# Softmax weights times v in three fp32r passes, divisors inverted in transposed 32x32 blocks, and a new order of the engines in attention

## The reference

```python
q_bits = (q @ proj > 0); k_bits = (k @ proj > 0)        # 6 bits per token
mask   = q_bucket[:, :, :, None] == k_bucket[:, :, None, :]
scores = where(mask, q @ k.T / 8, -1e9);  scores -= scores.max(-1)
attn   = exp(scores);  attn = attn / (attn.sum(-1) + 1e-9)
x = (attn @ v) as [1536, 512]
h = maximum(x @ w_in, 0);  x = h * h @ w_out            # 512 -> 2048 -> 512
# routing: tokens to 8 experts, 192 each, by descending logits of x @ w_gate
out[chosen by e] = maximum(x @ w1[e], 0) @ w2[e]        # 512 -> 1024 -> 512
```

## Time and profile before

| | us |
|---|---|
| median of 3 executions | 868.71 (867.45 to 880.04) |
| the profiled execution | 874.02 |
| its span, first to last instruction | 872.3 |
| attention in it, about | 24 to 309 |
| first layer | 309 to 590 |
| routing and experts | 590 to 872 |

### The profile page before, as it was taken

How to read it: one execution, slowest core, us unless ns; L and a number is a source line. 1 busy time by engine, 2 the same in 40 slices (tenths; PEclk the granted TensorE clock), 3 DMA queues, 4 the chain that set the end, 5 groups by cost and what they waited for, 6 DMA issues and landing times. The chain is left out here.

```text
span 872.3 us, 13757 instructions
## 1 busy us (share of the span) xinstructions
PE 816.2 (94%) x4688; PEld 703.0 (81%) x4688; DVE 416.4 (48%) x885; ACT 321.6 (37%) x575; POOL 283.4 (32%) x284
## 2 busy tenths in 40 slices
PE   5999999999999999999999999995399899999996
PEld 3776777767776778899989989994299899999996
DVE  7566666666666565242232224223644354455410
ACT  1344434444344555454554554440012122122221
POOL 3122312223122367655665566651100201110101
PEclk8899999999999999999999999996589999999999
DMA  7355546667545200010000001000344443635451
GB/s 170 73 116 117 126 91 131 139 144 173 136 96 138 88 1 0 0 37 1 0 36 0 0 0 37 0 1 36 115 150 159 166 178 129 217 134 208 136 208 36
DMA packets 65763, 81.28 MB, mean 93 GB/s; under 512 B 41304, under 2 KB 41304, under 8 KB 65216
## 3 DMA queue, kind: packets, MB, share of 16 engines
q1 hardware_dynamic: 63680, 74.54, 31.2%
q0 software_dynamic: 2048, 6.29, 2.2%
HBM read 54.55 MB, written 6.29 MB: 70 GB/s over the span
## 5 line engine op out<-in xcount | busy, mean ns | idle before, releaser
L586 PE MATMUL banks<-pt,v_raw 128*128 128x384 f32 x384 | 150.6, 489 | 0.0
L324 ACT ACTIVATE pt<-banks 128x768 f32<-128x768 f32 x96 | 77.9, 812 | 139.7 <-PE banks L536 138.5
L887 DVE TENSOR_TENSOR h<-relu 128x384 f32<-128x384 f32 x64 | 42.9, 670 | 174.0 <-ACT relu L842 174.0
L728 POOL TENSOR_TENSOR wi_lo<-w_in_sb,wi_hi 128x512 fp32r<-128x512 f32 x64 | 83.9, 1312 | 102.7 <-ACT wi_hi L721 101.6
L408 DVE TENSOR_REDUCE mx<-banks 128x1 f32<-128x768 f32 x96 | 91.7, 957 | 26.2 <-PE banks L563 23.3
L1406 PE MATMUL banks<-x_cols,w_in_sb 128*128 128x192 f32 x512 | 97.3, 343 | 1.3 <-ACT x_cols L1186 1.1
L1420 PE MATMUL banks<-expert_hidden,w_out_sb 128*128 128x192 f32 x512 | 94.6, 335 | 0.0
L732 POOL TENSOR_TENSOR wo_lo<-w_out_sb,wo_hi 128x512 fp32r<-128x512 f32 x64 | 84.7, 1323 | 15.1 <-ACT wo_hi L724 15.1
L1406 PEld LDWEIGHTS banks<-x_cols,w_in_sb 128*128 128x128 f32 x512 | 85.9, 198 | 3.8 <-issue 2.1
L962 PE MATMUL banks<-xt_hi,wi_hi 128*128 128x384 f32 (+1 forms) x256 | 86.4, 337 | 0.0
L962 PE MATMUL banks<-xt_lo,wi_hi 128*128 128x384 f32 (+1 forms) x256 | 86.0, 336 | 0.0
(11 more groups left out here) (181 smaller groups left out, 1288.7 us busy)
## 6 DMA issues: line engine op xcount, KB each, us to landing
w_in_sb<-in_moe_w SPq DMA_DIRECT2D x8, 2048.0 KB, 9.7
w_out_sb<-in_moe_w SPq DMA_DIRECT2D x8, 2048.0 KB, 8.1
w_in_sb<-in_moe_w_in SPq DMA_DIRECT2D x8, 512.0 KB, 6.1
w_out_sb<-in_moe_w_out SPq DMA_DIRECT2D x8, 512.0 KB, 5.1
w_out_sb<-in_k SPq DMA_DIRECT2D x16, 192.0 KB, 3.8
w_out_sb<-in_q SPq DMA_DIRECT2D x16, 192.0 KB, 3.9
v_raw<-in_v SPq DMA_DIRECT2D x16, 192.0 KB, 3.7
kb<-k_hi SPq DMA_DIRECT2D x16, 192.0 KB
```

The lines of the kernel that those rows point to most:

```text
L324: act.activation(halves(pt[j % 2]), both(ST), ACT.Exp, scale=SCALE).then_inc(ex, 1)
L586: last = pe.matmul(O[:, h, 0:HALF], v_raw[i][:, j, :], pt[j % 2][:, h * HALF:(h + 1) * HALF], start=False, stop=j == 5)
L728: pool.tensor_tensor(wil[i][:], in_view(f), wih[i][:].bitcast(fp32), ALU.subtract).then_inc(wils, 1)
```

## The change

- `weighted` goes. ScalarE makes pt_hi (fp32r) from pt in SBUF (`expo_high`), VectorE or GpSimd make pt_lo = pt - pt_hi (`low_part`: tiles 0 to 3 of the even head and 0, 1, 3 of the odd one on GpSimd, the other five on VectorE). v is split the same way (`v_high` on ScalarE, `v_low_part` on GpSimd). TensorE does v_hi x pt_hi, v_lo x pt_hi (`weigh_high`) and v_hi x pt_lo (`weigh_low`), each in fp32r for both halves.
- VectorE takes O out of PSUM whole (`take`, two halves), turns the divisor rows to the other partitions with a transpose in 32x32 blocks (`turn`), inverts one column per block (128x24) and spreads it by a second transpose (`invert`). GpSimd's `divide` is two operations of 64x768.
- The orders of all five engines are new; expo(j) waits for the low part that was read from its buffer, not for a matmul. v is loaded without padding and later; the weight loads of two heads stand together; GpSimd's first three weight splits stand behind the last divide.
- k_hi and the like share their memory with the weight splits of the first layer. The four reciprocals in the first chunk of that layer go.

```diff
-        v_raw = [sb(f"v_raw{i}", [P, TT, P]) for i in range(2)]
+        v_raw = [sb(f"v_raw{i}", [P, TT, D]) for i in range(2)]
+        def low_part(eng, i, p, j):
+            n = 2 * p + i
+            eng.wait_ge(his, 6 * n + j + 1)
+            if past(6 * n + j, 2):
+                eng.wait_ge(pvl, 6 * n + j - 1)
+            eng.tensor_tensor(pt_lo[j % 2][:], pt[j % 2][:], pt_hi[j % 2][:].bitcast(fp32), ALU.subtract).then_inc(los[i][j], 1)
...
SyncE, per pair:
+                asm_kb(2 * p + 1, 1)
+                part_ka(1)
+                asm_qb(2 * p + 1, 1)
+                part_qa(1)
+                more_q(p + 2)
+                if p + 1 < PAIRS:
+                    load_v(2 * p + 2, 0)
+                if p:
+                    load_v(2 * p + 1, 1)
+                weights(2 * p)
+                weights(2 * p + 1)
+                if p + 1 < PAIRS:
+                    asm_kb(2 * p + 2, 0)
+                    asm_qb(2 * p + 2, 0)
+                more_k(p + 2)
+                if p + 1 < PAIRS:
+                    part_ka(0)
+                    part_qa(0)
...
GpSimd:
             def divide(g):
                 pool.drain()
-                pool.wait_ge(num_, 2 * g + 1)
+                pool.wait_ge(evac, 4 * g + 2)
+                pool.wait_ge(rec, g + 1)
+                for i in range(2):
+                    pool.drain()
+                    pool.tensor_tensor(rden[VSL[i], :], nd[i][VSL[i], :], rden[VSL[i], :], ALU.mult).then_inc(nrm, 1)
...
+            for p in range(PAIRS):
+                if p:
+                    free_row(2 * p - 1, 1)
+                low_part(pool, 0, p, 0)
+                low_part(pool, 0, p, 1)
+                low_part(pool, 0, p, 2)
+                sum_v(2 * p + 1, 1)
+                low_part(pool, 0, p, 3)
+                if p:
+                    low(p - 1)
+                if p + 1 < PAIRS:
+                    free_row(2 * p, 0)
+                    sum_v(2 * p + 2, 0)
+                v_low_part(2 * p + 1, 1)
+                low_part(pool, 1, p, 0)
+                low_part(pool, 1, p, 1)
+                low_part(pool, 1, p, 3)
+                divide(p)
+                if p + 1 < PAIRS:
+                    v_low_part(2 * p + 2, 0)
+            split["in_low"](pool, 0, 0, 0)
+            split["in_low"](pool, 1, 1, 1)
+            split["out_low"](pool, 0, 0, 0)
             low(PAIRS - 1)
...
ScalarE:
             def expo(n, j):
                 act.wait_ge(st, 6 * n + j + 1)
+                if j > 1:
+                    act.wait_ge(los[n % 2][j - 2], n // 2 + 1)
+                elif n:
+                    act.wait_ge(los[(n - 1) % 2][j + 4], (n - 1) // 2 + 1)
+            def expo_high(n, j):
+                act.wait_ge(ex, 6 * n + j + 1)
                 if 6 * n + j > 1:
+                    act.wait_ge(pvh, 6 * n + j - 1)
+                act.activation(pt_hi[j % 2][:], pt[j % 2][:], ACT.Copy).then_inc(his, 1)
...
VectorE:
+            def take(n, i, h, divided):
+                dve.wait_ge(pvh, 6 * n + 6)
+                dve.wait_ge(pvl, 6 * n + 6)
                 if past(divided, 1):
                     dve.wait_ge(nrm, 2 * divided)
+                dve.tensor_copy(nd[i][:, h * HALF:(h + 1) * HALF], O[:, h, 0:HALF]).then_inc(evac, 1)
+            def turn(n, i):
+                dve.wait_ge(evac, 2 * n + 2)
+                dve.transpose(turned[VSL[i], :], nd[i][VSL[1 - i], :])
+            def invert(rows, free, done):
+                dve.drain()
+                dve.tensor_scalar(divisor[rows, :], turned[rows, :].rearrange("p (b c) -> p b c", c=SQ)[:, :, 0], GUARD, None, ALU.add)
+                dve.drain()
+                dve.reciprocal(divisor[rows, :], divisor[rows, :])
+                dve.drain()
+                dve.transpose(rden[rows, :].rearrange("p (b c) -> p b c", c=SQ),
+                              divisor[rows, :].unsqueeze(2).broadcast_to([rows.stop - rows.start, S // SQ, SQ])).then_inc(done, 1)
+            def pair(p, first, last):
+                if not first:
+                    low_part(dve, 1, p - 1, 5)
+                    take(2 * p - 1, 1, 0, p)
+                    take(2 * p - 1, 1, 1, p)
...
+                max_done(2 * p + 1)
+                low_part(dve, 0, p, 4)
+                if not first:
+                    turn(2 * p - 1, 1)
+                low_part(dve, 0, p, 5)
+                v_low(2 * p + 1, 1)
+                take(2 * p, 0, 0, p)
+                take(2 * p, 0, 1, p)
+                    row_max(2 * p + 2, 0)
+                turn(2 * p, 0)
+                    row_max(2 * p + 2, 1)
+                    row_max(2 * p + 2, 2)
+                    row_max(2 * p + 2, 3)
+                low_part(dve, 1, p, 2)
+                    row_max(2 * p + 2, 4)
+                    row_max(2 * p + 2, 5)
+                    max_done(2 * p + 2)
+                invert(EVERY, p, rec)
+                low_part(dve, 1, p, 4)
+                    v_low(2 * p + 2, 0)
...
TensorE (the new order of one pair, shortened; s_t = scores_t, s = scores of the next head):
+            def weigh_high(i, p, j):
+                if j == 0:
+                    pe.wait_ge(vls, n + 1)
+                pe.wait_ge(his, 6 * n + j + 1)
+                for v_ in (v_hi[i], v_lo[i]):
+                    for h in range(2):
+                        last = pe.matmul(O[:, h, 0:HALF], v_[:, j, :], pt_hi[j % 2][:, h * HALF:(h + 1) * HALF], start=False, stop=False)
+                last.then_inc(pvh, 1)
+            def weigh_low(i, p, j):
+                pe.wait_ge(los[i][j], p + 1)
...
```

501 lines of the change are left out of this document (253 added, 248 removed).

## The result

The changed kernel takes 885.26 us (median of 4 executions, 883.35 to 886.46) against 868.82 (4 executions) before: a ratio of 1.0155, 95% interval 1.0082 to 1.0228. I had predicted 858 with a range of 840 to 882; it is slower, by 0.8 to 2.3 per cent, and outside the range. The two profiled executions have spans of 881.6 and 872.3 us, 9.3 us apart. The medians are 16.4 us apart. The traces can explain the 9.3. The mean granted clock goes with this spread: of 82 executions of the kernel before on the four chips of the experiments, those under 870 us have clocks of 0.964 to 0.971 and those over 874.5 us 0.958 to 0.962; the profiled one has 0.961. So before's trace is that of an execution with a low clock.

The account below looks back on a forecast made before the run. TensorE was taken to bound the eight attention pairs. Seven pairs -11.5, last pair -1.5, hand-over +2, copies +1 and start +0.3 gave about -10 us, so 858 from the median of 868.7, range 840 to 882.

Parts of the forecast that it names:

- Pairs 2 to 7: Steady attention pairs: 34.6 us each instead of 36.25, predicted as -9.9 us for these six.
- the start: Start of the kernel, ahead of the first pair: four memsets for two, +0.3 us.
- The saving of the three passes: TensorE, per pair: 72 fp32r matmuls replace 24 fp32 ones, 2.9 us less, stream from 33.7 to 30.8 us.
- the first rival: Only TensorE and q count; GpSimd's divide and lows slip into idle time: pair 33.3 us, whole 849; chance 0.33.
- The chain ahead of scores_t(even, 3): First half of a pair: 12.4 us of GpSimd-led work beside 9.0 of TensorE; stall 2.9 us after overlap.
- The second half of the pair: Waits of 0.4 us at the next head's scores and 0.6 at weigh_low(even, 5): 1.0 us.
- The port rival: VectorE's low_parts each wait for a whole GpSimd operation: pair 40.1 us, whole 897; chance 0.14.
- The last pair: Last attention pair, without preparation: chain near 2 us per tile, gives back 1.5 of 30.0 us.
- The hand-over: Attention to first layer: in_low stands behind the last divide, about 2.5 us late, costing 2 us.
- The copies: kb and qb copies by SyncE: hidden but tight, 0 to 3 us in the whole, taken as +1.
- The clock: TensorE's lower busy share lowers its clock; a tenth of the stream at 1.2 GHz adds 25 us: 883; chance 0.05.
- ScalarE, VectorE and GpSimd: Work per pair: from 15.7, 24.4 and 9.1 us to 25, 27.9 and 26.

Follow-up runs that it names:

- without contention and divide: Changed kernel, divide on 32 of 768 columns, GpSimd's other attention reads replaced by memsets, odd head's weight copies at the pair's end: 850.19 us, 0.9763.
- The thin divide: Changed kernel with only 32 of 768 columns divided, the rest of the quotient left out: 870.62 us, 0.9978 of the kernel before.
- The best kernel: Changed kernel with VectorE taking numerators, ScalarE denominators, and most order edits; GpSimd's `low` in its old place: 862.12 us, 0.9898 of the kernel before.
- the seven memsets: Changed kernel with GpSimd's seven low_part per pair replaced by memsets of nearly equal length: 878.68 us, 1.0097 of the kernel before.
- the weight copies are moved: Changed kernel with the odd head's weight copies issued at the end of the pair; alone 881.11 us, 1.0125 of the kernel before.
- odd half first: Changed kernel with v_low_part and free_row ahead of divide, and the odd head divided first: 879.47 us, 1.0104 of the kernel before.
- hand-over: Changed kernel with the first layer's three first weight splits moved ahead of the last divide's end, around low_part(1,3): 883.22 us, 1.0146.
- last scores early: Changed kernel with the last pair's odd-head scores 0 to 3 in the places of the missing preparation: 884.47 us, 1.0188.

## Why the prediction was wrong

**Where the 19 us are.** I had -10 and the traces have +9.3. Pairs 2 to 7 missed by 12.7 us and the last pair with the hand-over by 10; the first pair (2.5) and the rest (1.7) came out better than I had them, the start 0.5 worse.

**The saving of the three passes: right.** I had 2.9 us per pair from the earlier trace rows. The fp32r matmuls of the new products follow each other at 0.174 us, and without contention and divide a pair takes 32.9 us (30.8 of stream by my count, and 2.1 besides). That is the 33.3 of the first rival: its size was right, its condition (GpSimd's work slips into idle time) was not met.

**The chain ahead of scores_t(even, 3): near, with a slip.** 9.97 us against 9.4 at that point. I had put the stall there as one wait of 2.9 us; it is 2.4, ahead of weigh_low and fallback, and z_q adds none of its own. My list had z_k and z_q at 0.52 us each, but each is six matmuls, 1.05 us. With them the list is 10.1 us long instead of 9.0 and the stall by my own chain 1.8 instead of 2.9; the point stays at 9.4. As the stream of 30.8 holds them in full, the slip put 1.1 us too much into the pair: without it I would have said 33.5, and missed by more. The thin divide shows that most of this stall is the divide's.

**The second half of the pair: the term that failed.** I gave it 1.0 us. From scores_t(even, 3) to the end of weigh_low(even, 5) it has 3.1, among them 0.9 before `rows` and 1.35 before weigh_low(even, 5); the odd head's half has 0.5 more. The step was the sentence "Now there are five per pair", on the earlier trace rows: I counted the VectorE operations with two SBUF inputs, found five pt_lo, and gave each 0.6 us. pt_lo measured 1357 ns, 0.4 more than 0.96, so that number was on the high side. But the one-input `has` and `mn` are held as well, and they are in the path. Nor was VectorE free of two SBUF inputs before: the first operation that writes `mn` (128x6, 168 ns) reads two. The kernel before has the hint: its own `mn` (128x12) has a mean of 412 ns, while `has` of half the size takes 173; where it takes 0.72, at 223.85, it stood behind GpSimd's memset of 223.81 already. My argument used neither group.

The runs give the price: contention 2.8 us, divide 1.9, together 3.9 of 36.8. The steady pair then is 32.9 + 3.9, and not 34.6.

**My own list, gone through with the rival's bound.** The port rival wanted 38.6 us per pair for +2%; the pairs stopped at 36.8. In the steady pairs its mechanism was the larger of the two, at half its price (2.8 us against 5.5), and it had 0.14. It should have had more, because the evidence of the earlier trace rows showed standstill for whole instructions, and I let "VectorE only has five" weigh against it without a look at what else VectorE reads from SBUF.

**The last pair: the second term that failed.** I wrote that it gives back 1.5 us of 30.0, by a chain of 2 us per tile and the saved stream. It takes 8 us more (41.58 - 31.03 - 2.48 of hand-over). TensorE's gaps, waits summed over 278.1 to 318.9 (engine, for whom: us in total, times, longest), and three timeline rows:

```profile
PEld banks L668 <- ACT pt L407: 3.6, 4, 1.8
PEld banks L727 <- DVE pt_lo L146: 2.5, 3, 1.3
PEld banks L727 <- POOL pt_lo L146: 2.2, 2, 1.4
```

```profile
289.20 5.81 DVE L511 TENSOR_REDUCE mx<-banks 128x1 f32<-128x768 f32 x6 [5.29 <-PE banks L696]
...
318.84 0.44 PE L1091 MATMUL banks<-xt_hi,split_parts 128*128 128x384 f32 x1 [2.48 <-POOL split_parts L861]
```

VectorE stands idle 5.3 us before the last head's maxima: the order of a full pair is kept, so the scores come after the chain of the divide although nothing else fills TensorE. That order is not the cause by itself, though: the even half lasts 21.8 us (row copies at 277.26 and 299.09) against 16.0 before (277.84 and 293.86), and with the divide thin and the other reads away, in the same order, it is back at 16.4. So nearly all of it is the same two causes as in a steady pair, which cost 5.5 us here in half a pair, as no preparation work fills TensorE meanwhile. Of the 10.55 us of last pair and hand-over, these causes hold 8.1, the hand-over's wait among them. I had costed this pair as a lighter steady pair, with nothing for the divide. The best kernel brings it to 35.1 us with the hand-over.

**The hand-over: size right.** +2 predicted, 2.48 of wait measured. That an earlier start wins nothing here (h_lo is late next) I had not seen.

**The copies: right that they are tight.** I took +1; it was 1.9 in one pair (37.1 us, and 35.2 without the wait). They are the next limit: `scores` waits 1.8 to 5.8 us for kb in one pair of six of the kernels whose pairs are shorter (in that of the seven memsets, 0.4), and not at all where the weight copies are moved.

**The clock** rival didn't occur in the steady pairs or the last one of the changed kernel: 1.00 from 28 to 316 us. But the clock moved the first pair (above), and in the experiments it fell behind the longer waits. **ScalarE, VectorE and GpSimd** were sized at 25, 27.9 and 26 us a pair and measured 24.6, 31.05 and 25.9; VectorE's excess of 3.1 is no more than its standing still, 5 x 0.4 for pt_lo and 2 x 1.0 for `has`. That GpSimd agrees is luck: my 26 hold 1.8 of drains, which don't count as busy, and the 25.9 hold 0.9 in which the divide stood still. The transposes cost 0.97, as taken.

What stays open: where in before's profiled execution its low clock lies; why the clock rises at 26.7 us in one kernel and at 32.6 in another; and the 2.1 us beyond the stream in the kernel without contention and divide.

## What to carry to other kernels

When work is added to VectorE and GpSimd together, list every VectorE operation that reads SBUF, small ones and one-input ones too, and ask which GpSimd instruction its start falls into; an operation of 0.17 us in the critical path can cost 1.3. Cost the first and the last turn of a pipelined loop by themselves: in the last one a chain has no other work to hide under. Look at the clock before the gain of a first turn is put down to the edit. And if a saving on the bounding engine is 2.9 us per turn, try the order with the suspected work thinned out first, since the floor (32.9 here) tells whether the rest is worth mending.

## What the runs showed of the hardware

**What GpSimd holds on VectorE.** A TENSOR_SCALAR with one SBUF input (128x6 or 128x12) stands still until the running GpSimd instruction ends, whether that reads (0.17 becomes 1.27 us) or is a memset (0.17 becomes 0.70). One of 128x24 takes 183 ns in the changed kernel and 777 in the best one. A TENSOR_TENSOR with two SBUF inputs stands still behind a reading one only (up to 2.30 for 0.96): started inside a memset it took its 0.96. The 32x32 transpose between SBUF tensors (0.97 us beside reads, for example 152.03) and maxima and copies out of PSUM are not held. GpSimd is held in turn (the divide takes 2.30 to 2.35 us, and the same form takes 1.86 in the kernel with both cuts, behind attention). The Trainium skill, "SBUF — State Buffer", section "SBUF: two separate sides", names exactly two kinds of VectorE operation that take the shared pair, those in a 2-port performance mode and those with two SBUF inputs, the latter only against a GpSimd operation that reads SBUF. The traces agree with the second half. They agree with the first if these TENSOR_SCALAR ran in such a mode, which no trace shows. I had used the second half and skipped the first.

**The clock after a gap.** In the changed kernel TensorE had 1.5 us of work in the 4 us before 320, and then got 0.57 of full speed, between the levels of 1.2 and 2.4 GHz, at full load:

```profile
316.00:320.00 4.00, 1.51 (x9) 1.20 (x9) 2.40 (x4) 0.84 (x1) 3.84 (x4) 1.00 0.01 4
320.00:324.00 4.00, 4.00 (x16) 4.00 (x16) 0.80 (x3) 1.99 (x4) 3.48 (x4) 0.57 0.01 2
```

From 324 to 332 us it had 0.79. At full load at most 3 us are lost by this (an estimate from the busy times and the clock of these 12 us). All that follows attention is not longer than in before's profiled execution (-0.7 us), but that execution had a low clock of its own, so the sum doesn't show that the fall was free.

**The clock after longer waits.** Behind 5.5 us without work it was 0.50 for 4 us (odd half first, 228 to 232), behind 6.0 us 0.50 from 324 to 328 (hand-over), behind 2.64 us 0.75 (last scores early, 284 to 288). Behind 1.69 us, in the changed kernel at 229, it stayed at 1.00.
